# Where the operands of TensorE lie in SBUF: other start residues within a 128-byte line

## The chip, the cores and the metric

The kernel runs on one core of one Trainium2 chip. The metric is the device time of one execution in microseconds. Three executions of the kernel before took 2348.56, 2346.13 and 2347.56 us; the median is 2347.56 us. Shorter is better.

## The reference

Three stages follow one another on 3072 tokens (4 batches of 768) with 384 features (8 heads of 48).

```python
# 1. attention: a delta-rule recurrence over time, per batch and head
y[:, :, t] = einsum('bhd,bhde->bhe', q[:, :, t], state)
v_old = einsum('bhde,bhd->bhe', state, kt)
state = state + bt * einsum('bhd,bhe->bhde', kt, vt - v_old)
# 2. first layer: 8 experts, all of them for every token
P = exp(x @ w_gate - max); 8 rounds of row and column normalisation
for e in range(8):
    out += P[:, e:e+1] * (relu(x @ w1[e]) @ w2[e])     # 384 -> 1024 -> 384
# 3. second layer
h = x @ w_in                                            # 384 -> 2048
return (h * cos(h)) @ w_out                             # 2048 -> 384
```

All arrays are float32.

## The kernel before, in words

The attention is computed in chunks of 64 steps, with many small matmuls. It fills the first 400 us or so; in it, parts of the first layer (the pass of expert 0's first half over five of six token tiles) are laid between the small matmuls. After that come the two layers alone.

In the layers a float32 operand is split in two: `hi` is the value rounded to the type `float32r`, `lo` is the rest. A product is then three matmuls that add into the same PSUM bank: hi times hi, hi weight times lo data, lo weight times hi data. In a matmul one operand is stationary (loaded into the array by LDWEIGHTS, here always 128x128 of a weight buffer `whi` or `wlo`), the other is moving (128x512, from `xhi`, `xlo`, `hhi` or `hlo`; it streams past).

A token tile has 512 tokens, so there are six. A pass is 512 hidden features: 16 passes for the eight experts (each in two halves) and 4 for the second layer. Passes alternate between two pairs of weight buffers, `whi0`/`wlo0` for the first half of an expert and `whi1`/`wlo1` for the second. For one tile of one pass TensorE does:

- `up`, for each of four chunks j of 128 hidden features: 3 x 3 matmuls (features d = 0 to 2, and the three products), moving `xhi`, `xlo`, `xhi`, stationary `whi`, `whi`, `wlo`, into bank `h` or `p_h`;
- ScalarE makes `hhi` of it (relu and rounding), VectorE makes `hlo`;
- `mm2` (the down product), for each j: 3 x 3 matmuls into three output banks, moving `hhi`, `hlo`, `hhi`, stationary `whi`, `whi`, `wlo` (second layer: `down2`, in the order `hhi`, `hhi`, `hlo`).

The order in a tile is up 0, up 1, down 0, up 2, down 1, up 3, down 2, down 3: 72 matmuls. In the first layer 91 tiles of this kind stand in the main part (one of the first pass, 15 x 6 of the others), and the second layer has 4 x 6 = 24 more: 115 x 72 = 8280 matmuls, half of them up, half down. The other tiles of the first pass, 5 x 72 = 360 matmuls, are those laid into the attention (lines 446 to 448 and 473 to 475), beside six groups of nine gate matmuls (`early_gate`, lines 455 to 457), whose stationary operand `wgr` has 8 columns only.

The order of work on every engine is written out by hand in program order with semaphores; no scheduler or planner decides anything. The buffers' addresses are set in `build` (lines 66 to 110) by `place`, which puts each buffer at the next multiple of 32 bytes behind the one before. All operands of the layers are addressed in steps of 512 bytes or its multiples within their buffers, so the residue of a buffer's start modulo 128 is that of all operands in it. In the kernel before, the residues work out as follows (address modulo 128): `hhi` and `hlo` 0; `whi0`, `wlo0`, `xhi`, `xlo`, `whi1`, `wlo1` all 32; the gate weights `wgr` start at 96, and their pieces (64 bytes for each d, 32 for hi and 32 for lo) have 96 and 0 for d = 0, 32 and 64 for d = 1, 96 and 0 for d = 2. Attention buffers share the space of `xhi`, `xlo`, `whi1`, `wlo1` and `scr`, which is why `x_at`, `xlo_at`, `w1_at` and `scr_at` are remembered.

Of the kernel before, what the change touches and what calls it, by code (L numbers as in the profile page):

```python
# [30 lines left out]

RAW, SUMMED, FIRST, WEIGHED = range(4)
EPS = 1e-9

INV_2PI = float(1.0 / (2.0 * np.pi))
SPLITS = (3, 6)
# [23 lines left out]
def build(nc, kta, kqt, krow, vrow, brow, wcat, wgate, out):  # L60
# [5 lines left out]
    at = [nc.sbuf_base]  # L66

    def place(name, shape, dt=F32, offset=None):
        size = 4 * int(np.prod(shape[1:]))
        if offset is None:  # L70
            offset = at[0]
            at[0] += (size + 31) // 32 * 32
        return nc.alloc_sbuf_tensor_at(name, shape, dt, offset=offset)

    def inside(base, name, shape, dt=F32):

        offset = base[0]
        base[0] += 4 * int(np.prod(shape[1:]))
        return nc.alloc_sbuf_tensor_at(name, shape, dt, offset=offset)
# [2 lines left out]
    at[0] = (at[0] + 31) // 32 * 32  # L82
    acc = place("acc", [P, DC, N_TOK])
    stage = place("stage", [P, WCOL])
    hhi = place("hhi", [P, CH, TILE], F32R)
    hlo = place("hlo", [P, CH, TILE], F32R)
    wgs = place("wgs", [P, DC, N_EXP])
    wgr = place("wgr", [P, DC, 2, N_EXP], F32R)
# [4 lines left out]
    halfpi = place("halfpi", [P, 1])  # L93
    ident8 = place("ident8", [P, N_EXP])

    whi0 = place("whi0", [P, WCOL], F32R)
    wlo0 = place("wlo0", [P, WCOL], F32R)
    x_at = at[0]
    xhi = place("xhi", [P, NT, DC, TILE], F32R)
    xlo_at = at[0]  # L100
    xlo = place("xlo", [P, NT, DC, TILE], F32R)
    w1_at = at[0]
    whi1 = place("whi1", [P, WCOL], F32R)
    wlo1 = place("wlo1", [P, WCOL], F32R)
    scr_at = at[0]
    scr = place("scr", [P, 3, 2, TILE])
# [5 lines left out]

    r = [w1_at]
    A_ = inside(r, "A_", [P, 2, U, CT])
    kT = inside(r, "kT", [P, U, CT])
    assert r[0] <= scr_at

    r = [scr_at]
    kq = inside(r, "kq", [P, KQ, HEADS, 2, CT])
    kb = inside(r, "kb", [P, STEPS, HEADS, HD])  # L120
    P_ = inside(r, "P_", [P, 2, HEADS, CT])
# [986 lines left out]
    def _(dve):  # L1108
# [212 lines left out]
        def row_sums(i, link):  # L1321
            link(dve.tensor_reduce(rs[:, :], prob[:, :, :], AX.X, ALU.add))
            link(dve.tensor_scalar(rs[:, :], rs[:, :], EPS, None, ALU.add))
            link(dve.reciprocal(rs[:, :], rs[:, :]))
# [3 lines left out]
        def columns(i, k, link):  # L1328
            dve.wait_ge(s["col_done"], i + 1)
            link(dve.tensor_scalar(cs[:, 1, :], yps[1 - k][0][:, 0:N_EXP], EPS, None, ALU.add))  # L1330
            link(dve.reciprocal(cs[:, 1, :], cs[:, 1, :]))
# [135 lines left out]
def program(nc, kta, kqt, krow, vrow, brow, wcat, wgate, out):  # L1467
    with build(nc, kta, kqt, krow, vrow, brow, wcat, wgate, out):
        pass
# [41 lines left out]
```

## Time and profile before

| | |
|---|---|
| median of three executions | 2347.56 us |
| the profiled execution: its own time | 2351.72 us |
| its span from first to last instruction | 2350.0 us |
| TensorE matmul busy | 2256.2 us (96%), 15460 instructions |
| weight loads busy | 1845.5 us (79%) |
| VectorE, ScalarE, GpSimd busy | 43%, 32%, 29% |
| chain that ended last | 75% matmuls, 12% issue, GpSimd 6%, VectorE 4%, ScalarE 2% |

In the profile a matmul's busy time counts from its start to its modelled end, and neighbours overlap: one that is listed with 0.39 or 0.40 us starts 0.23 us after the one before. The distance between starts is therefore what a matmul costs in a stream, and the busy share only says that the stream has no holes. A stretch's count of matmuls divided into its length gives that distance exactly; the single starts in a timeline are rounded to 0.01 us, so they are read over many matmuls.

### The profile page before, as it was taken

To read this page: it belongs to the slowest core of one execution; us is meant where nothing else is said; L and a number is where in the kernel's file an instruction comes from. 1 tells how busy PE (TensorE), PEld (TensorE's weight loads), DVE (VectorE), ACT (ScalarE), POOL (GpSimd) and SP (SyncE) were. 2 spreads that over 40 slices of the span, in tenths; PEclk is the share of its full clock that TensorE was granted. 3 is DMA by queue.
4 is the path that set the end of the run, shared out by engine and by line. 5 is a ranking of instruction groups with operands and counts; after the bars stand their busy time and mean duration, and the time that the engine had idled before them with its cause. 6 is when DMAs were issued, how large, how long until landed. Compare 5 with 4: busy or idle time off the path is not lost.

```text
span 2350.0 us, 40688 instructions
## 1 busy us (share of the span) xinstructions
PE 2256.2 (96%) x15460; PEld 1845.5 (79%) x15460; DVE 1012.5 (43%) x1621; ACT 741.9 (32%) x1288; POOL 686.6 (29%) x504
## 2 busy tenths in 40 slices
PE   3699998999999999999999999999999999999998
PEld 2688886788888888888888888888888877778786
DVE  4876742543232223232323223222323246777676
ACT  5555643311111111111111111111111226666665
POOL 3100001003523333232323232333323244444433
PEclk6689999999999999999999999999999999999999
DMA  5243332202101110111111011111111100000001
GB/s 157 71 116 96 88 95 79 94 14 65 40 27 32 27 45 27 31 27 31 29 43 30 28 31 27 34 37 31 27 31 27 45 22 14 14 14 14 0 14 67
DMA packets 85221, 102.35 MB, mean 44 GB/s; under 512 B 8384, under 2 KB 70144, under 8 KB 85120
## 3 DMA queue, kind: packets, MB, share of 16 engines
q1 hardware_dynamic: 85120, 100.91, 15.5%
q8 instruction: 75, 1.23, 0.2%
q14 instruction: 26, 0.21, 0.0%
HBM read 87.40 MB, written 8.75 MB: 41 GB/s over the span
## 4 chain that ended last, share of the span: by engine, by line
PE 75%; issue 12%; POOL 6%; DVE 4%; ACT 2%; SPq 1%; POOLq 0%; DMA 0%; DVEq 0%; ACTq 0%
PE h L595 5%; PE h L596 5%; PE p_h L595 5%; PE h L597 5%; PE p_h L597 5%; PE p_h L596 5%; POOL hlo L1102 4%; PE am_y L626 4%; PE am_y L624 4%; PE am_y L625 4%; PE chain_y L624 2%; PE chain_y L625 2%; PE chain_y L626 2%; PE o_y L624 2%; PE o_y L625 2%
## 5 line engine op out<-in xcount | busy, mean ns | idle before, releaser
L1081 POOL TENSOR_TENSOR acc<-acc,py 128x512 f32 (+1 forms) x252 | 325.3, 1319 | 760.8 <-DVE py L1385 760.8
L945 ACT ACTIVATE hhi<-h 128x512 fp32r<-128x512 f32 x182 | 109.1, 599 | 790.4 <-PE h L597 790.4
L1352 DVE SCALAR_TENSOR_TENSOR hlo<-h,hhi 128x512 fp32r<-128x512 f32 x182 | 125.9, 692 | 483.9 <-ACT hhi L945 483.9
L1352 DVE SCALAR_TENSOR_TENSOR hlo<-p_h,hhi 128x512 fp32r<-128x512 f32 x182 | 125.9, 692 | 411.7 <-ACT hhi L945 411.7
L1049 POOL TENSOR_TENSOR wlo<-stage,whi (+1 forms) x114 | 156.8, 1377 | 448.7 <-ACT whi L835 423.1
L595 PE MATMUL h<-xhi,whi 128*128 (+1 forms) x690 | 271.1, 393 | 2.4 <-DVE scr L1453 2.4
L596 PE MATMUL h<-xlo,whi 128*128 (+1 forms) x690 | 270.0, 391 | 0.0
L595 PE MATMUL p_h<-xhi,whi 128*128 (+1 forms) x690 | 269.9, 391 | 0.0
L597 PE MATMUL h<-xhi,wlo 128*128 (+1 forms) x690 | 268.7, 389 | 0.0
L597 PE MATMUL p_h<-xhi,wlo 128*128 (+1 forms) x690 | 268.5, 389 | 0.0
L596 PE MATMUL p_h<-xlo,whi 128*128 (+1 forms) x690 | 268.5, 389 | 0.0
L945 ACT ACTIVATE hhi<-p_h 128x512 fp32r<-128x512 f32 x182 | 109.0, 599 | 440.4 <-PE p_h L597 440.4
L1102 POOL TENSOR_TENSOR hlo<-scr,hhi 128x512 fp32r<-128x512 f32 x96 | 142.0, 1479 | 231.7 <-ACT hhi L983 231.7
L595 PEld LDWEIGHTS h<-xhi,whi 128*128 128x128 f32 x690 | 129.8, 188 | 33.2 <-issue 3.6
L595 PEld LDWEIGHTS p_h<-xhi,whi 128*128 128x128 f32 x690 | 129.5, 188 | 29.1 <-DVE scr L1453 1.7
L597 PEld LDWEIGHTS h<-xhi,wlo 128*128 128x128 f32 x690 | 129.9, 188 | 28.6
L596 PEld LDWEIGHTS h<-xlo,whi 128*128 128x128 f32 x690 | 129.9, 188 | 28.4
L597 PEld LDWEIGHTS p_h<-xhi,wlo 128*128 128x128 f32 x690 | 129.5, 188 | 27.7
L596 PEld LDWEIGHTS p_h<-xlo,whi 128*128 128x128 f32 x690 | 129.6, 188 | 27.3
L626 PE MATMUL am_y<-hhi,wlo 128*128 128x512 f32 x368 | 145.5, 396 | 0.0
L625 PE MATMUL am_y<-hlo,whi 128*128 128x512 f32 x368 | 145.5, 395 | 0.0
L624 PE MATMUL am_y<-hhi,whi 128*128 128x512 f32 x368 | 145.5, 395 | 0.0
(223 smaller groups left out, 4109.7 us busy)
## 6 DMA issues: line engine op xcount, KB each, us to landing
stage<-wcat SPq DMA_DIRECT2D x40, 768.0 KB, 4.3
pb<-p_scratch SPq DMA_DIRECT2D x84, 256.0 KB, 4.7
kq<-kqt SPq DMA_DIRECT2D x48, 192.0 KB, 3.4
kn<-krow SPq DMA_DIRECT2D x6, 768.0 KB, 5.5
kT<-kta SPq DMA_DIRECT2D x24, 192.0 KB, 5.3
v<-vrow SPq DMA_DIRECT2D x24, 192.0 KB, 3.9
kb<-krow SPq DMA_DIRECT2D x24, 192.0 KB, 4.9
out<-acc SPq DMA_DIRECT2D x6, 768.0 KB, 3.8
```

The lines of the kernel that those rows point to most:

```text
L595: pe.matmul(hps[bank][:, 0:TILE], w1(whi, buf, d, j), x_h, start=(d == 0), stop=False)
L596: pe.matmul(hps[bank][:, 0:TILE], w1(whi, buf, d, j), x_l, start=False, stop=False)
L597: mm = pe.matmul(hps[bank][:, 0:TILE], w1(wlo, buf, d, j), x_h, start=False, stop=(d == DC - 1))
L624: pe.matmul(y, w2(whi, half, j, d), hhi[:, j, :], start=(j == 0), stop=False)
L625: pe.matmul(y, w2(whi, half, j, d), hlo[:, j, :], start=False, stop=False)
L626: mm = pe.matmul(y, w2(wlo, half, j, d), hhi[:, j, :], start=False, stop=(j == CH - 1))
L945: act.activation(hhi[:, j, :], hps[j % 2][:, 0:TILE], ACT.Relu).then_inc(s["hhi_done"], 1)
L1049: pool.tensor_tensor(wlo[buf][:, c], stage[:, c], whi[buf][:, c].bitcast(F32), ALU.subtract).then_inc(s["wlo_done"], 1)
L1081: pool.tensor_tensor(y, y, py[:, d, :], ALU.add).then_inc(s["added"], 1)
L1102: pool.tensor_tensor(hlo[:, j, :], gg[:, j % 2, :], hhi[:, j, :].bitcast(F32), ALU.subtract).then_inc(s["h2_split"], 1)
L1352: dve.scalar_tensor_tensor(out=hlo[:, j, :], in0=hps[j % 2][:, 0:TILE], scalar=0.0, in1=hhi[:, j, :].bitcast(F32), op0=ALU.max, op1=ALU.su ...
```

## The change

A helper `line(residue)` moves the address at which the next buffer is placed forward to the next one with the given residue modulo 128. It is called ahead of each buffer of the layers that TensorE reads. The buffers' sizes, their order, all instructions and their order on every engine stay as they are; the start addresses of everything behind `stage` grow by 32 to 256 bytes.

```diff
+LINE = 128
...
+    def line(residue):
+
+        at[0] += (residue - at[0]) % LINE
+        return at[0]
...
     stage = place("stage", [P, WCOL])
+    line(32)
     hhi = place("hhi", [P, CH, TILE], F32R)
+    line(64)
     hlo = place("hlo", [P, CH, TILE], F32R)
     wgs = place("wgs", [P, DC, N_EXP])
...
+    line(0)
     whi0 = place("whi0", [P, WCOL], F32R)
+    line(64)
     wlo0 = place("wlo0", [P, WCOL], F32R)
-    x_at = at[0]
+    x_at = line(0)
     xhi = place("xhi", [P, NT, DC, TILE], F32R)
-    xlo_at = at[0]
+    xlo_at = line(32)
     xlo = place("xlo", [P, NT, DC, TILE], F32R)
-    w1_at = at[0]
+    w1_at = line(32)
     whi1 = place("whi1", [P, WCOL], F32R)
+    line(32)
     wlo1 = place("wlo1", [P, WCOL], F32R)
     scr_at = at[0]
```

| buffer | role | residue before | residue after |
|---|---|---|---|
| `whi0`, `wlo0` | stationary, first halves | 32, 32 | 0, 64 |
| `whi1`, `wlo1` | stationary, second halves | 32, 32 | 32, 32 |
| `xhi`, `xlo` | moving, up | 32, 32 | 0, 32 |
| `hhi`, `hlo` | moving, down | 0, 0 | 32, 64 |
| `wgr` | stationary, gate | 96 | 32 |
| `scr`, `pb`, `py`, `A_`, `kT`, `kq`, `kb`, `v`, `R`, `W`, `S` | other engines, attention | 32 | 32 |
| `X`, `kn`, `a_leaf` (in the space of `xhi`) | attention | 32 | 0 |

## Rows read from the trace of the kernel before

**Rows 1.** Stretches: busy us and count by engine, then granted clock.
```profile
core 0: us, PE busy (x) PEld busy (x) DVE busy (x) ACT busy (x) POOL busy (x), PEclk, DMA share, GB/s
600.00:1800.00 1200.00, 1200.00 (x5206) 977.30 (x5205) 350.56 (x507) 210.60 (x361) 374.36 (x295) 1.00 0.12 32
1850.00:2350.00 500.00, 486.71 (x2087) 390.70 (x2086) 318.56 (x402) 268.19 (x433) 207.71 (x137) 0.99 0.06 21
```

**Rows 2.** Groups by line and shape: busy us, mean ns; idle before, releaser.
```profile
L595 PE MATMUL h<-xhi,whi 128*128 x600 | 235.7, 393 | 2.4 <-DVE scr L1453 2.4
L596 PE MATMUL p_h<-xlo,whi 128*128 x600 | 233.4, 389 | 0.0
L625 PE MATMUL am_y<-hlo,whi 128*128 128x512 f32 x368 | 145.5, 395 | 0.0
L624 PE MATMUL o_y<-hhi,whi 128*128 128x512 f32 x180 | 71.7, 398 | 0.0
```

**Rows 3.** Timeline, TensorE: start us, length, line; an up product's steady part.
```profile
904.77 0.39 PE L595 MATMUL h<-xhi,whi 128*128 x1
904.99 0.39 PE L596 MATMUL h<-xlo,whi 128*128 x1
...
907.49 0.40 PE L624 MATMUL o_y<-hhi,whi 128*128 128x512 f32 x1
```

**Rows 4.** Timeline, TensorE: a down product, first matmul to the next up's.
```profile
911.63 0.40 PE L624 MATMUL o_y<-hhi,whi 128*128 128x512 f32 x1
911.87 0.40 PE L625 MATMUL o_y<-hlo,whi 128*128 128x512 f32 x1
...
913.73 0.40 PE L595 MATMUL p_h<-xhi,whi 128*128 x1
```

**Rows 5.** Timeline, TensorE: an up product's first five, after a down product.
```profile
903.38 0.39 PE L595 MATMUL h<-xhi,whi 128*128 x1
...
904.54 0.39 PE L597 MATMUL h<-xhi,wlo 128*128 x1
```

**Rows 6.** Timeline, TensorE: a group of nine gate matmuls at full clock.
```profile
394.60 0.40 PE L455 MATMUL o_y<-xhi,wgr 128*8 128x512 f32 x1
...
395.07 0.39 PE L457 MATMUL o_y<-xhi,wgr 128*8 128x512 f32 x1
395.29 0.40 PE L455 MATMUL o_y<-xhi,wgr 128*8 128x512 f32 x1
395.53 0.40 PE L456 MATMUL o_y<-xlo,wgr 128*8 128x512 f32 x1
...
396.45 0.39 PE L457 MATMUL o_y<-xhi,wgr 128*8 128x512 f32 x1
```

**Rows 7.** Weight loads: of the gate (min/median/max ns) and of the layers.
```profile
L455 PEld LDWEIGHTS o_y<-xhi,wgr x18: 86/88/130, 185.1 to 417.6; 128*8 128x8 f32 x18
...
L596 PEld LDWEIGHTS h<-xlo,whi 128*128 128x128 f32 x690 | 129.9, 188 | 28.4
```

**Rows 8.** Timeline, TensorE, and its stretch: gate matmuls at the lower clock.
```profile
416.28 0.63 PE L457 MATMUL o_y<-xhi,wgr 128*8 128x512 f32 x1
...
417.99 0.63 PE L455 MATMUL o_y<-xhi,wgr 128*8 128x512 f32 x1
...
410.00:418.50 8.50, 3.04 (x8) 0.96 (x9) 1.76 (x1) 1.48 (x1) 0.00 (x0) 0.61 0.80 281
```

**Rows 9.** Groups of VectorE: input residues 0 and 32.
```profile
L1352 DVE SCALAR_TENSOR_TENSOR hlo<-h,hhi 128x512 fp32r<-128x512 f32 x182 | 125.9, 692 | 483.9 <-ACT hhi L945 483.9
L1385 DVE TENSOR_TENSOR py<-am_y,pb 128x512 f32<-128x512 f32 x84 | 57.8, 692 | 1.2 <-issue 0.4
```

**Rows 10.** All waits of TensorE between 1850 and 2350 us: total, times, longest.
```profile
PE chain_y L693 <- POOL hlo L1102: 5.2, 8, 2.2
PE h L595 <- DVE scr L1453: 2.4, 1, 2.4
```

## The prediction

> **What bounds the kernel now.** I read the busy time by stretch first. Between 600 and 1800 us TensorE is busy for all of 1200 us at a granted clock of 1.00 (that is 2.4 GHz), with 5206 matmuls: one every 1200 / 5206 = 230.5 ns. In the second layer it is busy for 486.7 of 500 us [rows 1]. The groups by line say why nothing else counts there: the matmuls have next to no idle time before them [rows 2], and in the last 500 us the listed waits of TensorE sum to 7.6 us [rows 10]. VectorE has some 350 us of work in those 1200, GpSimd 374, ScalarE 211 [rows 1]. So from about 430 us on the time is a count of matmuls times the distance between their starts, and the only thing that a change of addresses can move is that distance, or a duration on another engine that is hidden anyway.
>
> Then the timeline, because the mean durations hint at two kinds: 389 to 393 ns for up matmuls, 395 to 398 for down [rows 2]. These lengths overlap and are not the cost; the starts are. Twelve starts of an up product from 904.77 to 907.49 give 2.72 / 12 = 226.7 ns [rows 3]. Nine of a down product from 911.63 to 913.73 give 2.10 / 9 = 233.3 ns [rows 4]. 512 columns at 2.4 GHz are 213.3 ns, so an up matmul carries 13.3 ns more than its columns and a down matmul 20.0. In between lies a transition: the first five up matmuls after a down product take 904.54 - 903.38 = 1.16 us, or 232.0 ns each, before the stream finds its 226.7 [rows 5]. It is TensorE's stream alone that does this. At the lower clock the gate matmuls are 0.427 us apart (416.28 to 417.99, four of them, where the stretch's granted clock averages 0.61 [rows 8]), which is 512 columns at 1.2 GHz with nothing added.
>
> What differs between up and down is the residue: up has stationary and moving operand both at 32, down has the stationary at 32 and the moving at 0. The third sample is the gate: moving at 32, stationary at 96, 0, 32 and 64 in turn. Its eight starts from 394.60 to 396.45 are 1.85 / 8 = 231.3 ns apart, with one of 0.22 us among them (395.07 to 395.29) and the others 0.23 to 0.24 [rows 6]. Its weight loads take 88 ns, those of the layers 188 [rows 7], and still the matmuls are not closer. So the length of the load isn't what costs; the start addresses may be, through both operands.
>
> The Trainium skill says otherwise. "TensorE: Matmul & The Clock Gate", section "Back-to-back issue gap", gives N / 2.4 + 2.5 ns at full clock, about 216 ns for 512 columns, with no word on addresses, and its Part 2 says that loading the next weights takes no read bandwidth from a running matmul. The trace disagrees with the first: 226.7 ns at best in a steady stream.
>
> **The change part by part.** No instruction is added, removed or reordered. What moves:
>
> Layers, 8280 matmuls in the main part. By stationary and moving residue, in the order hi-hi, lo data, lo weight, they are now: first halves up (0,0) (0,32) (64,0), down (0,32) (0,64) (64,32); second halves up (32,0) (32,32) (32,0), down (32,32) (32,64) (32,32). Before, each stream of nine had one residue on the moving side and one on the stationary; now the moving residue changes twice in every three matmuls. Only the difference 0 with nothing else changing has ever shown 226.7, and it needs a steady run to get there. Such runs are gone in both halves. What stands in the trace for mixed streams is the gate (231.3) and the transition (232.0). Bounds from both sides: below, all 8280 at the up rate, 226.7 - 230.5 = -3.8 ns each, -31 us; above, the down rate or a little over, 235 ns (the 0.24 us ends of single distances in [rows 6] lie about there), +4.5 ns each, +37 us. I take 232.0, the transition's, and not 231.3, as here the moving residue changes too, which in the gate it doesn't: +1.5 ns x 8280 = +12.4 us.
>
> The 360 matmuls laid into the attention and the gates: the same +1.5 ns on 360 is 0.5 us, and part of these hide behind the attention's waits. Bounds by the same two rates: -1.4 to +1.6 us. I take 0.
>
> Small matmuls of the attention: of their operands only `X` moves in residue (32 to 0), a stationary operand of 64 columns. There are 24 chunks x 16 = 384 of these. At the 6.6 ns between the two kinds of [rows 3, 4] the bounds are -3 to +3 us; I take 0, as I have no sample for small ones and part of them hides behind waits.
>
> Other engines: VectorE's operation on `hhi` at residue 0 takes 692 ns, that on `pb` at residue 32 takes 692 ns as well [rows 9]. No effect; and if one came, VectorE has 1200 - 351 us of room in the stretch [rows 1]. In the second layer each step is a round of ScalarE, VectorE and GpSimd, where a slower operation would show at once as a wait like those of [rows 10]; since none slows, nothing is added. A slower TensorE there only shortens them.
>
> Sum: the profiled execution took 2351.72 us; + 12.4 gives 2364.1. It ran 4.2 us above the median of the three, so for the median: 2347.6 + 12.4 = 2360.0 us, slower by 0.5%.
>
> **The rivals.**
>
> The moving operand's own residue decides, and 0 is the bad one (down before: moving 0, slow; up: moving 32, fast). For it: it fits both layer streams. Against: the gate's moving operand lies at 32 and its stream is at 231.3 [rows 6]. After the change `xlo`, `hhi` and `hlo` are off 0, 48 of 72 matmuls in a tile, and `xhi` is on it, 24 of 72: (48 x 226.7 + 24 x 233.3) / 72 = 228.9 ns, -1.6 ns x 8280 = -13 us: 2334 us. A stronger form: alternating residues let the next matmul begin in a nearer slot, as the gate's 0.22 us distance may show, and the whole stream falls to 226.7 or under: -31 us, 2316 us. This is the side on which the forecast would be wrong in sign, and it decides from a mean distance under 230 ns.
>
> The number of pairs at equal residue decides and nothing else. What runs at one time is a moving stream and the load of the next matmul's weights. First halves of the first layer: up, two of three at equal residue; down, one. Second halves: one and two. That is 36 of 72 in nearly all tiles, as before (all up, no down). The sum is 0 to +1 us: 2348 us. Counted by a matmul's own two operands instead, 12 of 72 are equal in the first halves and 36 in the second, (55 x 12 + 60 x 36) = 2820 against 4140 before, 1320 matmuls at +6.6 ns, +9 us: this lies with the forecast.
>
> The change does nothing, as the difference between up and down is one of output banks (up stays in a bank for nine matmuls, down for three). Against: the gate stays in one bank for nine and has 231.3 [rows 6]. 2348 us as well. By the Trainium skill, "SBUF — State Buffer", section "Specifications (TRN2)", which gives lines of 16 bytes, a shift by 32 or 64 bytes leaves every operand equally aligned, and nothing should move; up and down before differ by 32 bytes and by 6.6 ns, which speaks against it, though not by itself.
>
> Every mixed pair is worse than the transition: all at 235 ns, +37 us, 2385 us. For it: residue 64 on the moving side has no sample in the trace.
>
> **How the numbers follow.** Forecast, 2354 to 2370 us: 0.41. Every pair worse, to 2385: 0.06. No change by the count of pairs or because addresses don't matter: 0.15. Faster by the moving residue, about 2334: 0.26; faster by nearer slots, down to 2316: 0.12. What a measurement can tell from no change here is about 0.2%, or 4.7 us. So faster 0.38, same 0.15, slower 0.47. Some 2 in 10 may stay outside: I cut the far half of the 2316 case and the 2385 case, which gives 2323 to 2376. The forecast's own range is 2354 to 2370.
>
> **What would show it.** The count of matmuls between 600 and 1800 us: 5172 at 232.0 ns if I am right, 5206 if nothing changed, 5242 at 228.9. In the timeline, up products should have lost their even 226.7; down products should lie near 232. First and second halves of an expert should differ if residues of pairs matter, and be alike if only the moving side does. VectorE at 692 ns and ScalarE's relu unchanged. The forecast fails if a mixed stream settles into a rhythm closer than 230 ns.

## The result and the profile after

The changed kernel takes 2357.66 us (median of three, 2356.84 to 2358.92) against 2347.56 us before: +10.1 us, a ratio of 1.0041 with a 95% interval of 1.0027 to 1.0055. It is slower by 0.4%. The forecast was 2360.0 us.

The first view is the busy time by stretch of the changed kernel, the answer to [rows 1] (busy us and count for TensorE, weight loads, VectorE, ScalarE, GpSimd; then granted clock, DMA share, GB/s):

```profile
600.00:1800.00 1200.00, 1200.00 (x5178) 971.45 (x5177) 346.75 (x502) 209.62 (x360) 371.93 (x293) 1.00 0.12 32
1850.00:2350.00 500.00, 492.75 (x2093) 393.73 (x2091) 320.09 (x403) 268.07 (x433) 208.26 (x137) 0.99 0.06 20
```

In the 1200 us TensorE is as full as before, at the same clock, but it starts 5178 matmuls and not 5206: 231.7 ns each and not 230.5. It waits no more than before: 6.7 us in the last 500 us against 7.6 in [rows 10]. The others wait a little longer for its results, ScalarE 792.8 us against 790.4 ahead of its relu on `h`. TensorE's waits in the last 500 us, and VectorE's operations, beside [rows 9]:

```profile
PE chain_y L704 <- POOL hlo L1113: 4.4, 4, 2.1
PE h L606 <- DVE scr L1464: 2.3, 1, 2.3
```

```profile
L1363 DVE SCALAR_TENSOR_TENSOR hlo<-h,hhi 128x512 fp32r<-128x512 f32 x182 | 125.9, 692 | 489.2 <-ACT hhi L956 489.2
...
L1396 DVE TENSOR_TENSOR py<-am_y,pb 128x512 f32<-128x512 f32 x84 | 57.8, 691 | 0.8 <-issue 0.4
```

The timeline of TensorE shows what the average hides (start us, length, line; lines 606 to 608 are the up product's, 635 to 637 the down product's). First half of an expert, an up product and a down product:

```profile
955.77 0.40 PE L606 MATMUL h<-xhi,whi 128*128 x1
...
957.85 0.40 PE L635 MATMUL chain_y<-hhi,whi 128*128 128x512 f32 x1
...
959.93 0.40 PE L606 MATMUL p_h<-xhi,whi 128*128 x1
```

And of a second half:

```profile
1051.68 0.40 PE L606 MATMUL p_h<-xhi,whi 128*128 x1
...
1053.78 0.40 PE L635 MATMUL chain_y<-hhi,whi 128*128 128x512 f32 x1
...
1055.86 0.40 PE L606 MATMUL h<-xhi,whi 128*128 x1
```

Nine distances each: first half up 2.08 / 9 = 231.1 ns, down 231.1; second half up 2.10 / 9 = 233.3, down 231.1. Up has lost its 226.7 ns of [rows 3], down has gained 2.2 ns on its 233.3 of [rows 4]. The mean over all distances under 250 ns between starts of the first layer says the same: up 227.7 before and 232.1 after, down 233.4 before and 231.6 after.

Where the microseconds went is read from the first start of the first layer's main part and that of the second layer. A line's own view gives them (duration min/median/max, first and last start). Before:

```profile
L595 PE MATMUL h<-xhi,whi x690: 389/389/787, 419.0 to 2330.9; 128*128 x150, 128*128 128x512 f32 x23
...
L693 PE MATMUL o_y<-hhi,whi x48: 397/397/494, 1941.7 to 2327.5; 128*128 128x512 f32 x48
```

After:

```profile
L606 PE MATMUL h<-xhi,whi x690: 387/397/629, 411.7 to 2336.1; 128*128 x150, 128*128 128x512 f32 x23
...
L704 PE MATMUL o_y<-hhi,whi x48: 389/397/629, 1943.8 to 2332.6; 128*128 128x512 f32 x48
```

| stretch, us | before | after |
|---|---|---|
| start of the first layer's main part | 419.0 | 411.7 |
| from there to the second layer's first down product | 1522.7 | 1532.1 |
| from there to the span's end (2350.0, 2355.1) | 408.3 | 411.3 |

The two layers together are 12.4 us longer. The attention ahead of them was 7.3 us shorter in this one execution, which is why the two spans differ by 5.1 us only. In it TensorE was granted a different clock, before and after (the last three numbers of a line are the granted clock, the DMA share and GB/s):

```profile
60.00:240.00 180.00, 153.09 (x3672) 138.04 (x3673) 138.79 (x312) 104.88 (x200) 21.76 (x4) 0.82 0.36 95
60.00:240.00 180.00, 152.24 (x3741) 137.36 (x3742) 139.05 (x313) 107.55 (x203) 21.76 (x4) 0.85 0.38 97
```

Over the fourteen profiled executions of this study the start of the main part lies anywhere from 408.7 to 419.6 us; the earliest had 0.87 in this stretch, the latest 0.79, and the earliest belongs to a kernel whose attention operands lie as in the kernel before (419.0 us, 0.82). So I compare the stretches behind it.

### The profile page after: what moved, and what is told of

It is laid out like the page before. It is cut to its first block, busy times and chain, and to the rows that moved or that the text cites. A ratio compares the mean times of both kernels' runs of the same rounds, so it can differ in the third digit from the quotient of the medians.

```text
span 2355.1 us, 40688 instructions
## 1 busy us (share of the span) xinstructions
PE 2263.0 (96%) x15460; PEld 1842.5 (78%) x15460; DVE 1013.2 (43%) x1621; ACT 741.4 (31%) x1288; POOL 685.9 (29%) x504
## 4 chain that ended last, share of the span: by engine, by line
PE 74%; issue 12%; POOL 6%; DVE 5%; ACT 2%; SPq 1%; POOLq 0%; DMA 0%; DVEq 0%; ACTq 0%
PE p_h L606 5%; PE h L606 5%; PE h L607 5%; PE p_h L607 5%; PE p_h L608 5%; PE h L608 5%; POOL hlo L1113 4%; PE am_y L636 4%; PE am_y L635 4%; PE am_y L637 4%; PE chain_y L635 2%; PE o_y L635 2%; PE chain_y L637 2%; PE chain_y L636 2%; PE y_y L636 2%
## 5 line engine op out<-in xcount | busy, mean ns | idle before, releaser
L956 ACT ACTIVATE hhi<-h 128x512 fp32r<-128x512 f32 x182 | 108.9, 598 | 792.8 <-PE h L608 792.8
```

Of the source, the lines that this page charges most:

```text
L956: act.activation(hhi[:, j, :], hps[j % 2][:, 0:TILE], ACT.Relu).then_inc(s["hhi_done"], 1)
```

## The experiments

All kernels are the changed one with other numbers in its `line(...)` calls (the last also moves two buffers' data); the edits are shown shortened. The measure beside the device time is the length of the first layer's stretch as in the table (1522.7 before, 1532.1 after) and the count of matmuls between 600 and 1800 us. Where two kernels have the same distances in all pairs, their stretches agree within 0.2 us (1523.7 and 1523.9, 1498.6 and 1498.7), and that is the yardstick for kernels with one execution only. From "All at 0 modulo 256" on residues are given modulo 256; the kernel before has then `hhi`, `hlo` 128 and all others 160; the changed one has `hhi` 160, `hlo` 192, `whi0` 0, `wlo0` 64, `xhi` 128, `xlo` 160, `whi1`, `wlo1` 160.

**All at 32, all at 0 (modulo 128).**

```diff
-    line(32)  # hhi
-    line(64)  # hlo
-    line(0)   # whi0
-    line(64)  # wlo0
-    x_at = line(0)
+    line(32)  # all eight; in the second kernel line(0)
+    x_at = line(32)
```

> All eight layer buffers (hhi, hlo, whi0, wlo0, xhi, xlo, whi1, wlo1) start at residue 32. Pair theory (a stream whose moving and stationary operands all have one residue runs at 226.7 ns a matmul): down products drop from 233.5 to 226.7 ns, 4140 x 6.8 = -28 us, and the transitions behind them go too, about -2 us: 2318 us. Moving-operand theory (its own residue decides, 32 good, 0 bad): the same 2318. Bank theory (down is slower because it changes banks every three matmuls): unchanged, 2348, down still at 233.3 ns.

> All eight at residue 0. Pair theory: equal residues again, 2318 us, up and down both at 226.7 ns. Moving-operand theory: every moving operand is at the bad residue 0, all 8280 at 233.3 ns, up products lose 4140 x 6 = +25 us against the kernel before: 2373 us. Bank theory: 2348.

Measured: 2349.31 us, ratio 1.0006 (0.9994 to 1.0019), and 2351.21 us, ratio 1.0011 (0.9998 to 1.0024). The stretches are 1523.7 and 1523.9 us. Both theories of mine fell in the form in which I had put them: neither 2318 nor 2373. An up and a down product of the first kernel:

```profile
957.24 0.39 PE L606 MATMUL p_h<-xhi,whi 128*128 x1
...
959.30 0.40 PE L635 MATMUL chain_y<-hhi,whi 128*128 128x512 f32 x1
...
961.40 0.39 PE L635 MATMUL chain_y<-hhi,whi 128*128 128x512 f32 x1
```

Down is at 2.10 / 9 = 233.3 ns though its operands have the same residue modulo 128 as its weights. Either output banks decide, or 128 is the wrong modulus.

**`hhi`, `hlo` at 96, the others at 32; and `xhi`, `xlo` at 0, the others at 32 (modulo 128).**

```diff
-    line(32)  # hhi
+    line(96)  # hhi, hlo; the others line(32)
```

> hhi and hlo at 96, all others at 32: the down pairs are 64 bytes apart. If the pattern repeats every 64 bytes, down runs as with equal residues, 226.7 ns, 2318 us. If it repeats only every 128 bytes, down is a mixed stream of another kind than 32 apart: between 230 and 235 ns, 2335 to 2353 us. Bank theory: 2348.

> xhi and xlo at 0, the weights and hhi, hlo at 32: the kernel before with the roles of up and down exchanged. Pair theory: up at 233.3 ns, down at 226.7, total as before within 3 us (2345 to 2351). Moving-operand theory: the same. Bank theory: up stays at 226.7 and down at 233.3.

Measured: 2353.97 us, ratio 1.0027 (1.0014 to 1.0040), down at 233.3 ns, as expected for a pattern of 128 bytes or for banks, the time 1 us over that range; and 2364.43 us in a single execution, with 5175 matmuls between 600 and 1800 us. None of the three theories had the second one, and it gave the key, in a second half of an expert:

```profile
1058.41 0.40 PE L606 MATMUL p_h<-xhi,whi 128*128 x1
...
1060.52 0.39 PE L635 MATMUL chain_y<-hhi,whi 128*128 128x512 f32 x1
...
1062.58 0.40 PE L606 MATMUL h<-xhi,whi 128*128 x1
1062.82 0.40 PE L607 MATMUL h<-xlo,whi 128*128 x1
...
1064.68 0.40 PE L635 MATMUL chain_y<-hhi,whi 128*128 128x512 f32 x1
```

Up 2.11 / 9 = 234.4 ns and 2.10 / 9 = 233.3, down 2.06 / 9 = 228.9 with the step in at its start. Up is slow in the banks in which it was fast, so it isn't the banks. And in this kernel down is fast in second halves and slow in first halves (227.7 against 233.2 ns over all down matmuls of the first layer), though modulo 128 `whi0` and `whi1` lie alike. Modulo 256 they don't: the paddings happen to put `whi0` at 32, `whi1` at 160 and `hhi` at 160. Five of the six kernels so far (all but the changed one, whose residues alternate within a stream) have one distance between moving and stationary residue in each stream. Where it is 0 modulo 256, the first layer's mean is 227.7 to 228.5 ns; where it is 96, 128, 192 or 224, it is 232.8 to 233.8 ns.

**All at 0 modulo 256.**

```diff
-LINE = 128
+LINE = 256
-    line(32)  # and so on
+    line(0)   # all eight
```

> All eight layer buffers at residue 0 modulo 256 instead of 128. Theory now (the pair's distance counts modulo 256): up and down both settle at 226.7 ns, transitions go: down 4140 x 6.8 = -28 us, up 4140 x 0.8 = -3 us against the kernel before: 2317 us. Rival (the first two tries with equal residues modulo 128 left down at 233 for another cause, such as its change of output bank every three matmuls): 2348 us, down at 233 ns.

Measured: 2314.45 us, ratio to the kernel before 0.9859 (0.9828 to 0.9890). This is faster than both kernels, by 33 and 43 us at the medians. Its stretch, its two starts, and a tile with an up and a down product:

```profile
600.00:1800.00 1200.00, 1200.00 (x5296) 993.78 (x5295) 353.40 (x514) 214.35 (x368) 379.89 (x299) 1.00 0.13 33
```

```profile
L606 PE MATMUL h<-xhi,whi x690: 387/389/791, 412.4 to 2293.9; 128*128 x150, 128*128 128x512 f32 x23
...
L704 PE MATMUL o_y<-hhi,whi x48: 389/389/490, 1911.0 to 2290.5; 128*128 128x512 f32 x48
```

```profile
1035.57 0.39 PE L606 MATMUL h<-xhi,whi 128*128 x1
...
1037.61 0.39 PE L606 MATMUL p_h<-xhi,whi 128*128 x1
...
1039.65 0.39 PE L635 MATMUL chain_y<-hhi,whi 128*128 128x512 f32 x1
...
1041.69 0.39 PE L606 MATMUL h<-xhi,whi 128*128 x1
```

Each nine take 2.04 us, 226.7 ns, up and down, with no step in between, whatever the output bank. 1200 us / 5296 = 226.6 ns. The first layer's stretch is 1498.6 us (24.1 less than before), the second layer's 401.5 (6.8 less).

**The weights that load meanwhile, or a matmul's own.**

```diff
+LINE = 256: hhi, whi0, xhi 128; hlo, wlo0, xlo, whi1, wlo1 192
```

> Modulo 256: whi0, xhi, hhi at 128; wlo0, xlo, hlo, whi1, wlo1 at 192. In the first layer's first halves each moving operand then has the residue of the weights that are loaded while it streams (those of the next matmul), but only one of three has that of its own weights. If what runs at one time decides: 226.7 ns in first halves. If a matmul's own two operands decide: first halves mixed, 230 to 234 ns. Second halves are mixed in both, 230 to 234. Total 2330 to 2350 us by the first, 2350 to 2365 by the second.

That the next weights load while a matmul streams is read from the kernel before, where both start together (PEld is the weight load):

```profile
903.38 0.39 PE L595 MATMUL h<-xhi,whi 128*128 x1
903.38 0.19 PEld L596 LDWEIGHTS h<-xlo,whi 128*128 128x128 f32 x1
```

Measured in a single execution: 2367.41 us, above both of my ranges, with the longest stretch of all, 1538.7 us. In first halves nine distances of an up product take:

```profile
955.13 0.40 PE L606 MATMUL h<-xhi,whi 128*128 x1
...
957.21 0.40 PE L606 MATMUL p_h<-xhi,whi 128*128 x1
```

2.08 / 9 = 231.1 ns. Equal residues with the next matmul's weights alone are thus not enough. As the moving residue also changes from matmul to matmul there, the run doesn't show that a matmul's own pair is what decides; that stays open. Second halves are at 234.7 (up) and 234.2 ns (down) over the whole first layer, just over the range I had given.

**The two halves of the change apart.** The moving operands as in the changed kernel, weights as before; then the weights of first halves as in the changed kernel, the rest as before.

```diff
+LINE = 256: hhi 160, hlo 192, xhi 128, xlo 160; weights 160
+LINE = 256: whi0 0, wlo0 64; hhi, hlo 128; xhi, xlo, whi1, wlo1 160
```

> The moving half of the change alone, modulo 256: hhi 160, hlo 192, xhi 128, xlo 160 as in the changed kernel, all weights at 160 as before. One of three up matmuls and two of three down have equal residues; if only unbroken equal streams reach 226.7, up rises to 231 to 234 ns and down stays between 229 and 232: first-layer stretch 1520 to 1535 us long, against 1522.6 before and 1532.1 changed. If equal pairs count one by one with nothing lost between them, it is 1522 us at most.

> The stationary half of the change alone, modulo 256: whi0 0, wlo0 64, all others as in the kernel before (whi1, wlo1, xhi, xlo 160; hhi, hlo 128). Second halves then are those of the kernel before in every residue: up 226.7 to 228.5 ns, down 233.3. In first halves no pair is equal any more: up rises to 230 to 235 ns (1548 up matmuls x 5 = +8 us), down keeps its 231 to 235. First-layer stretch 1528 to 1535 us, against 1522.6 before.

Single executions: 2361.98 us, and 2346.96 us. First layer's stretch 1532.6 and 1525.1 us, where the changed kernel has 1532.1 and the one before 1522.7. Their counts between 600 and 1800 us:

```profile
600.00:1800.00 1200.00, 1200.00 (x5171) 970.20 (x5170) 347.82 (x504) 209.41 (x359) 372.85 (x294) 1.00 0.12 32
```

```profile
600.00:1800.00 1200.00, 1200.00 (x5197) 976.13 (x5196) 348.39 (x505) 210.07 (x360) 375.55 (x295) 1.00 0.12 32
```

The moving half alone costs all that the change costs in the first layer (+9.9 of +9.4 us), the stationary half alone 2.4 us, less than the 5 to 12 us that I had expected, and together they are not the sum: where up went from 227.7 to 231.3 ns in first halves, down came from 233.4 to 231.5. The device time of the second (2346.96, single) would have hidden that: its attention ended early (408.7 us), which is why the stretch is read.

The kernel with the moving half alone also answers whether 256 is the modulus or 512. Its `whi1` and `wlo1` lie 256 bytes off `whi0` and `wlo0` when counted modulo 512, and at the same place modulo 256. The starts of three passes in a row, a first half, a second and a first:

```profile
736.38 0.40 PE L606 MATMUL h<-xhi,whi 128*128 x1
...
836.66 0.40 PE L606 MATMUL h<-xhi,whi 128*128 x1
...
936.94 0.40 PE L606 MATMUL h<-xhi,whi 128*128 x1
```

Both halves take 100.28 us, and their means agree (up 232.9 ns, down 231.3 in either), so 256 bytes more or less change nothing in these streams. In the all-equal kernels all distances are 0 modulo 512 too, so for a full-rate stream this isn't tested in the same way.

**A scan of distances.**

```diff
+LINE = 256: hhi, hlo 160; whi0, wlo0 0; xhi, xlo 32; whi1, wlo1 224
```

> Modulo 256: hhi, hlo 160; whi0, wlo0 0; xhi, xlo 32; whi1, wlo1 224. Distances moving minus weights: up 32 in first halves, 64 in second; down 160 and 192. If every distance but 0 costs the same, all four streams lie at 233.3 ns (192 has been seen there): 4140 x 6 = +25 us, 2373 us. If some distance leaves TensorE undisturbed, one stream falls under 226.7.

Single execution: 2364.63 us, neither the 2373 us of four alike streams nor a stream under 226.7 ns. Means over all first-layer distances between starts under 250 ns: up 232.8 ns at distance 32, 229.2 at 64; down 233.9 at 160, 232.6 at 192. The rate at 64, in the timeline:

```profile
1056.29 0.39 PE L606 MATMUL h<-xhi,whi 128*128 x1
...
1058.35 0.39 PE L606 MATMUL p_h<-xhi,whi 128*128 x1
```

2.06 / 9 = 228.9 ns. So the distances aren't all alike, and none beats 0.

**One operand out of line, and 16 bytes.** All at 0 modulo 256 but `hlo` at 32; all at 160; and all at 128 but the second halves' weights begin 16 bytes further.

```diff
+LINE = 256, all line(0), but hlo: line(32)
+LINE = 256, all line(160)
+LINE = 256, all line(128); whi1, wlo1 of WCOL + 8 columns, used from column 4 on
```

> All at 0 modulo 256 but hlo at 32. If each matmul pays for its own pair, only the 12 of 72 with hlo rise, by 5 to 7 ns: 1092 in the first layer, +7 us on the 1498.6 us of all-equal. If one unequal operand spoils the stream around it, all 36 down matmuls of a tile rise by 3 to 7 ns and the first up matmuls behind them too: +12 to +24 us, 1511 to 1523 us. Up streams at 226.7 ns in both, but for their beginnings.

> All eight at 160 modulo 256, instead of 0. If only the distance within pairs matters, as with all at 0: 2314 us, first-layer stretch 1498 to 1500 us, ratio to the kernel before 0.986. If the absolute residue matters too, anything up to 2348.

> All eight at 128 modulo 256, but in second halves the weights' data begins 16 bytes further (distance moving minus stationary -16 bytes). First halves are all equal: 226.7 ns. If the distance must be 0 to the byte, second halves rise to 230 to 235 ns: 3456 matmuls x 5.5 = +19 us on the first layer's 1498.6. If 16 bytes lie within the same unit as 0, second halves stay at 226.7 and the stretch at 1499 us.

All at 160: 2314.39 us, ratio 0.9867 (0.9834 to 0.9900), the stretch 1498.7 us: the absolute residue doesn't matter. With `hlo` out of line, a single execution of 2358.50 us and a stretch of 1525.3 us, +26.7 us on all-equal and beyond even the upper end of my range. Two up products there, whose own operands all lie at 0: the second of the two that stand together at a tile's start, and one between down products:

```profile
1055.96 0.39 PE L606 MATMUL p_h<-xhi,whi 128*128 x1
...
1058.00 0.39 PE L635 MATMUL chain_y<-hhi,whi 128*128 128x512 f32 x1
...
1060.09 0.39 PE L606 MATMUL h<-xhi,whi 128*128 x1
...
1062.17 0.39 PE L635 MATMUL chain_y<-hhi,whi 128*128 128x512 f32 x1
```

The first is at 2.04 / 9 = 226.7 ns, the second at 2.08 / 9 = 231.1: a sixth of the matmuls lies out of line, and of a tile's eight products only one keeps the full rate (the up product at the tile's very start has 229.0 ns on average, the two between down products 231.2, down 232.0). With 16 bytes a single execution took 2323.11 us, the stretch 1499.8 us, and most second halves run at the full rate, up and down 2.04 us for nine:

```profile
1043.91 0.39 PE L606 MATMUL p_h<-xhi,whi 128*128 x1
...
1045.95 0.39 PE L635 MATMUL chain_y<-hhi,whi 128*128 128x512 f32 x1
...
1047.99 0.39 PE L606 MATMUL h<-xhi,whi 128*128 x1
```

So a distance of 16 bytes can cost as little as 0 does, but it doesn't hold there. The second layer is 405.3 us long against 401.5, and the trace shows why: in its last pass, which reads `whi1` and `wlo1`, all products run at the slow rate, from a matmul on that had to wait for `hlo` (the idle time before it and what ended it stand in brackets). The last line is the view by stretch:

```profile
2214.77 0.50 PE L704 MATMUL chain_y<-hhi,whi 128*128 128x512 f32 x1 [0.16 <-POOL hlo L1113]
...
2216.98 0.40 PE L606 MATMUL h<-xhi,whi 128*128 x1
...
2219.08 0.40 PE L704 MATMUL o_y<-hhi,whi 128*128 128x512 f32 x1
```

```profile
2215.00:2300.00 85.00, 85.00 (x365) 68.83 (x365) 60.06 (x77) 49.99 (x81) 29.45 (x20) 1.00 0.08 28
```

2.10 / 9 = 233.3 ns, and 85 / 365 = 232.9 ns up to 2300 us, at the same addresses and the same granted clock at which second halves of the first layer take 226.7. All-equal at 0 starts 376 matmuls in the same 85 us. No pass at distance 0, in this kernel or in the two all-equal ones, has such a stretch. Whether the 16 bytes make the rate unsteady isn't shown, for `wlo1` also came to lie 256 bytes off `wlo0` modulo 512 here.

## Why the prediction was right

**The frame held.** From 430 us on the time is a count of matmuls times the distance of their starts. No other engine came into it: VectorE at 692 and 691 ns, ScalarE's relu at 598 ns against 599, the waits of TensorE even shorter. The rival that a shift by 32 or 64 bytes does nothing is out: the same instructions ran from 226.6 to 232.7 ns a matmul between 600 and 1800 us (5296 and 5156 starts) on addresses alone. It was the Trainium skill's lines of 16 bytes ("SBUF — State Buffer", "Specifications (TRN2)") that supported it.

**The term of the sum.** I took 232.0 ns for mixed streams from the transition [rows 5]; measured 231.7, with 231.1 to 233.3 in the four streams. The counts I gave as signs were 5172 if right and 5206 if nothing changed; it is 5178. The term was +12.4 us, and the two layers are 12.4 us longer; the median moved by 10.1. The agreement to a tenth is luck: rates between 231 and 233 stood behind it, and the start of the layers varies by ten. That the transition's 232.0 ns is also what an alternating stream settles at had no ground but nearness; other alternating streams here average 231.1 to 234.7 ns, which would have been +5 to +35 us on 8280 matmuls.

**The step that was right for an incomplete reason.** I wrote that only distance 0 "has ever shown 226.7, and it needs a steady run to get there", and that such runs are gone in both halves. Both are shown, by all-equal at 0 and 160 and by the one operand out of line. But I read the distance modulo 128, as the change is written. It counts modulo 256. The pairs that I listed as equal in first halves, up (0,0) and the like, are 128 bytes apart, and with that first halves have no equal pair at all. It didn't hurt, since an equal pair in a mixed stream buys little: the changed kernel's first halves, with none, take 100.03 us a pass, its second halves, with 36 of 72, take 100.28. It would have hurt the moment I used it: it gave 2318 us for the first two experiments, which came out at 2349 and 2351.

**The bounds.** The lower one, all matmuls at the up rate, -31 us, is what all-equal modulo 256 reaches: its two layers are 30.9 us shorter (-33 by the medians). As a bound it was sound; as a fate of this change it was never near. One small bound was drawn too tight: I took 384 small matmuls with the stationary operand `X`, as the program has them, and the trace has two for each, 768, which at 6.6 ns makes 5 us and not 3. What they did can't be told from the attention's own spread.

**The rivals.** "The moving operand's own residue, 0 bad" fell with all at 0 modulo 256, which is the fastest kernel here. "Alternating residues let the next matmul begin in a nearer slot" fell with every alternating stream: in the changed kernel single distances go down to 223 ns, but no nine in a row took under 2.07 us, 230 ns each. "The number of equal pairs" fell with `hlo` out of line: 60 of 72 matmuls keep equal pairs and 26.7 us are lost. "Output banks" fell with `xhi` moved. "Every mixed pair at 235 ns" fell with the result; only one arrangement came near it, the second halves of the kernel for the next matmul's weights (234.7 and 234.2 ns).

## What to carry to other kernels

Where TensorE is the bound and streams 512 columns of float32r without holes, read the distance between matmul starts in each kind of stream before anything else. If two kinds differ by some 3% with nothing waiting, compare the start addresses of the moving and the stationary buffers modulo 256, not 128. Put all of them at one residue modulo 256: it cost 352 bytes of padding here and gave 1.4%. A last buffer that can't be aligned may take back the whole gain: with `hlo` alone 32 bytes off, the stretch is 1525.3 us, longer than the 1522.7 of the kernel before, in which all of down is off and all of up in line.

## What the runs showed that I had not expected

A stream with all distances 0 modulo 256 runs at 226.7 ns per 128x512 float32r matmul at 2.4 GHz, 13.3 ns above its 512 columns, and no arrangement went lower. "TensorE: Matmul & The Clock Gate" of the Trainium skill, section "Back-to-back issue gap", has about 216 ns for an isolated matmul and about 131 ns for a stream of weight loads and matmuls; no run here shows either. Streams with unequal distances average 229.2 to 234.7 ns in the first layer, by distance and by what mixes. What in the chip has the 256 bytes, and why the clock's lower level shows nothing of it (0.427 us for 512 columns in [rows 8]), no run here tells.

A sixth of the matmuls out of line costs as much as half: 1525.3 us with `hlo` alone at 32, 1523.7 with both `hhi` and `hlo` 128 bytes off. After an unequal stream, an equal one needs some matmuls to find its rate ([rows 5]), and what stands between counts: up products between down products average 227.3 ns in the kernel before, where all of down has one distance, and 231.2 with `hlo` alone out of line, where the distance alternates. Why an alternating neighbour costs more than a steady one stays open.
